# Two edits to a kernel of attention and two expert layers: a wait of the gathers of noise is left out, and one piece of TensorE's work is put behind a vote

## The reference

```
x  = attention(q, k, v)            # 4 x 8 heads x 768, chunks of 32 keys with 16 to the left, 8 to the right, 8 memory keys
x  = moe(x)                        # 3072 tokens, 8 experts, capacity 384 each

def _moe_ref(x, w_gate, w1, w2):
    logits = x @ w_gate
    order = np.argsort(-logits.flatten())
    for idx in order:              # the best (token, expert) pairs first
        tok, e = idx // E, idx % E
        if assigned[tok] >= 0 or counts[e] >= cap: continue
        assigned[tok] = e; counts[e] += 1
    for e in range(E):
        out[assigned == e] = relu(x[assigned == e] @ w1[e]) @ w2[e]

def _moe2_ref(x, w_gate, w_noise, noise, w1, w2):
    noisy = x @ w_gate + log1p(exp(x @ w_noise)) * noise
    # the best two experts of each token, weighted by the softmax of their two values
    # out += weight * (relu(x @ w1[e]) @ w2[e])
```

## Time and profile before

| | |
|---|---|
| median of 3 runs | 1321.05 us (1320.45 to 1321.9) |
| profiled execution, its own time | 1320.45 us |
| its span | 1318.6 us |
| TensorE's mean granted clock | 0.969 of full speed |
| busy, of the span | PE 93%, DVE 69%, ACT 43%, POOL 22% |

### The profile page before, as it was taken

How to read it: one execution, slowest core, us unless ns; L and a number is a source line. 1 busy time by engine, 2 the same in 40 slices (tenths; PEclk the granted TensorE clock), 3 DMA queues, 4 the chain that set the end, 5 groups by cost and what they waited for, 6 DMA issues and landing times.

```text
span 1318.6 us, 27799 instructions
## 1 busy us (share of the span) xinstructions
PE 1229.2 (93%) x9680; PEld 1094.3 (83%) x9680; DVE 915.5 (69%) x1818; ACT 572.2 (43%) x1224; POOL 291.1 (22%) x346
## 2 busy tenths in 40 slices
PE   6999983289999999999999999999999999999997
PEld 5888872278787787888898999989999898999986
DVE  4777765887887878765697666666666666766662
ACT  4666650123333233344415544544455444544541
POOL 4000000111211211220223323324233242333322
PEclk9999995589999999999999999999999999999999
DMA  8878744433331432543305233233333423334210
GB/s 147 167 169 166 167 100 175 152 113 108 126 121 64 146 128 73 176 156 121 110 28 198 72 106 111 81 104 106 126 122 121 144 79 104 100 125 135 88 43 13
DMA packets 174299, 154.65 MB, mean 117 GB/s; under 512 B 105118, under 2 KB 137886, under 8 KB 174241
## 3 DMA queue, kind: packets, MB, share of 16 engines
q1 hardware_dynamic: 151552, 102.83, 27.9%
q0 software_dynamic: 16128, 44.56, 10.9%
q10 hardware_dynamic: 6560, 6.49, 1.4%
HBM read 206.13 MB, written 33.75 MB: 182 GB/s over the span
## 4 chain that ended last, share of the span: by engine, by line
PE 38%; issue 36%; DVE 10%; POOL 9%; DMA 3%; ACT 2%; POOLq 1%; another core or an unknown queue 0%; SPq 0%; DVEq 0%; ACTq 0%
PE bank L792 8%; PE bank L772 8%; DMA out<-result,token_now 3%; POOL partial L424 3%; PE bank L648 3%; POOL out L434 3%; PE bank L657 2%; PE bank L636 2%; POOL held L404 2%; PE bank L1004 2%; PE bank L672 2%; POOL x L408 2%; PE bank L718 2%; PE bank L1031 2%; PE bank L757 1%
## 5 line engine op out<-in xcount | busy, mean ns | idle before, releaser
L575 DVE TENSOR_TENSOR w_part<-w_sb,w_part 128x1024 fp32r<-128x1024 f32 x280 | 341.6, 1223 | 98.0 <-ACT w_part L569 90.1
L569 ACT CAST w_part<-w_sb 128x1024 fp32r<-128x1024 f32 x280 | 290.6, 1046 | 205.9 <-PE bank L1031 152.5
L1004 PEld LDWEIGHTS bank<-x2T,w_part 128*128 128x128 f32 x2688 | 326.3, 192 | 4.4 <-DVE x2T L1561 1.4
L1004 PE MATMUL bank<-x2T,w_part 128*128 128x256 f32 x2688 | 327.9, 283 | 1.6 <-DVE x2T L1561 1.6
L1031 PE MATMUL bank<-w_part,h2T 128*128 128x512 f32 x1344 | 312.6, 391 | 0.0
L1031 PEld LDWEIGHTS bank<-w_part,h2T 128*128 128x128 f32 x1344 | 250.2, 188 | 51.0
L792 PE MATMUL bank<-w_part,hT 128*128 128x512 f32 x576 | 155.2, 406 | 3.7 <-DVE w_part L575 3.7
L772 PE MATMUL bank<-xgT,w_part 128*128 128x384 f32 x768 | 147.0, 344 | 0.9 <-DVE xgT L1225 0.9
L1916 ACT ACTIVATE h2T<-bank 128x512 fp32r<-128x512 f32 x112 | 66.9, 597 | 178.6 <-PE bank L1004 141.1
L772 PEld LDWEIGHTS bank<-xgT,w_part 128*128 128x128 f32 x768 | 134.1, 191 | 2.9 <-DVE xgT L1225 1.4
L1567 DVE SCALAR_TENSOR_TENSOR h2T<-bank,h2T 128x512 fp32r<-128x512 f32 x112 | 77.3, 690 | 79.9 <-ACT h2T L1916 55.8
(11 more groups left out here) (281 smaller groups left out, 1337.2 us busy)
## 6 DMA issues: line engine op xcount, KB each, us to landing
w_sb<-in_moe_w SPq DMA_DIRECT2D x280, 512.0 KB
k_in<-in_k SPq DMA_DIRECT2D x32, 240.0 KB
v_in<-in_v SPq DMA_DIRECT2D x32, 240.0 KB
q_in<-in_q SPq DMA_DIRECT2D x32, 192.0 KB
x_dram<-x_sb SPq DMA_DIRECT2D x32, 192.0 KB, 3.2
out<-zeros SPq DMA_DIRECT2D x1, 6144.0 KB, 19.7
y_dram<-y_sb ACTq DMA_DIRECT2D x24, 256.0 KB, 2.0
x<-y_dram,slot_now POOLq DMA_INDIRECT x56
```

What stands on the lines that cost most here:

```text
L569: scalar.copy(split_part(0, c), raw_part(c)).then_inc(hi_ready[c], 1)
L575: nc.vector.tensor_tensor(split_part(1, c), raw_part(c), split_part(0, c).bitcast(F32), ALU.subtract).then_inc(lo_ready[c], 1)
L1004: last = nc.tensor.matmul(bank[2 + g % 2][:, at:at + TILE], w1_part[a][:, kt, f * P:(f + 1) * P], x2T[b][:, kt, :], start=(f % 2 == 0 and ...
```

## The change

```diff
@@ -379,9 +379,6 @@
                     pool.indirect_dma_start(out=xg[:, c % TPE, :], out_offset=None, in_=x_dram[:, :],
                                             in_offset=bass.IndirectOffsetOnAxis(ap=token_of[:, c:c + 1], axis=0),
                                             bounds_check=N - 1, oob_is_err=False).then_inc(gathered[c % TPE], 16)
-                if e < E - 2:
-
-                    pool.wait_ge(s1_ready, e * FT + 6)
                 for c in range(e * TPE, (e + 1) * TPE):
                     pool.indirect_dma_start(out=noise_g[:, c, :], out_offset=None, in_=moe2_noise[:, :],
                                             in_offset=bass.IndirectOffsetOnAxis(ap=token_of[:, c:c + 1], axis=0),
@@ -806,8 +803,8 @@
 
             def step(n, k, j):
 
-                before_votes = (0, 6, 9, 12, 15, 20, 22)
-                after_votes = (3, 8, 11, 14, 17, 21, 24)
+                before_votes = (0, 6, 9, 12, 15, 18, 22)
+                after_votes = (3, 8, 11, 14, 17, 20, 24)
                 done = 0
                 for s in range(len(SHIFTS)):
                     count(n, s)
```

## The result

| | before | after |
|---|---|---|
| median, on the chip on which both were first timed | 1320.81 us (4 runs, 1320.45 to 1321.90) | 1329.26 us (4 runs, 1327.67 to 1332.73) |
| ratio, with its 95% interval | | 1.0063 [1.0047, 1.0079] |
| profiled execution, its span | 1320.45, 1318.6 us | 1327.07, 1325.2 us |
| TensorE's mean granted clock | 0.969 | 0.966 |

The kernel is slower by 0.6%, 8.4 us, where 1320.1 us and "no difference that can be told" were forecast. The time is outside the forecast's range (1318.0 to 1322.3), and a slower kernel was given 6%.

A forecast was written before the change was run, and what follows sets the result against it. VectorE was taken to set the pace early in each step, TensorE from 402.20 to 421.80 in step 4. Terms -0.96 + 0.05 + 0 = -0.9 us, from 1321.05 to 1320.1 us; range 1318.0 to 1322.3.

The forecast's parts named there:

- The second edit, gain: Combine pieces moved from ahead of vote 5 to ahead of vote 6: vote 5 earlier, vote 6 unmoved, gain 0.
- Rival A: VectorE's 2.25 us idle before vote 5 is on the path: 1.41 us gained in five steps, 1313.1 us; 8%.
- The second edit, cost: Vote 5 behind three matmuls instead of nine still comes 0.6 us after VectorE's comparison: no new wait, cost 0.
- The first edit, cost in steps 2 to 6: Noise gathers in their new place hold VectorE up by at most 0.3 us, hidden in its slack: cost 0.
- Rival B: The 0.28 us gap ahead of the first comparison is due to gathers: 1.1 us more gain, 1319.0 us; 7%.
- The first edit, gain: Noise gathers leaving each step's start free VectorE's small instructions, shortening TensorE's weight-block wait: 0.96 us over steps 2 to 6.
- Step 1: No combine there, VectorE on the path: moved gathers may hold up L1359, bounds 0 to 0.3 us, taken as 0.05.
- Rival C: First gathered block lands too late for the earlier transposes: up to 1.41 us lost in five steps, 1327.2 us; 6%.

The follow-up runs named there:

- E2: Kernel before with only the combine pieces moved, noise gathers waiting as before: 1320.17 us, ratio 1.0000.
- E9: Kernel before with only the combine pieces moved, repeated on another chip: 1320.64 us, ratio 1.0006.
- E16: Kernel before with only the combine pieces moved, repeated to mark the chip's kind: 1320.98 us, ratio 1.0006.
- E18: Kernel before with only the combine pieces moved, on a chip with late signals: 1321.88 us, ratio 1.0002.
- E17: Kernel before with only the noise gathers moved up behind those of xg, on a chip with late signals: 1319.17 us, ratio 0.9977.
- E6: Kernel before, unchanged, profiled on a chip without late signals: 1320.77 us, ratio 1.0002.
- E1: Kernel before with only the noise gathers moved up behind those of xg, combine pieces as before: 1318.84 us, ratio 0.9993.
- E5: Kernel after, unchanged, on a chip without late signals: 1319.55 us, ratio 0.9990.
- E14: Kernel after, unchanged, run as a marker of the chip's kind: 1320.02 us, one run.
- E7: Kernel after, unchanged, a third time on yet another chip, which showed late signals: 1327.39 us, ratio 1.0052.
- E4: Kernel after without the third noise gather of the first six expert places, that noise zero: 1320.12 us, ratio 0.9997.
- E13: Kernel before with only the noise gathers moved up behind those of xg, repeated: 1320.60 us, ratio 1.0002.
- E8: Kernel before with only the noise gathers moved up behind those of xg, repeated: 1319.00 us, ratio 0.9992.
- E11: Kernel after, noise gathers of six places replaced by 2 KB rows of x, their noise zero, repeated: 1367.15 us, ratio 1.0358.
- E12: Kernel before with only the noise gathers moved up behind those of xg, repeated: 1319.38 us, ratio 0.9989.
- E3: Kernel after, noise gathers of the first six places replaced by 2 KB rows of x, their noise zero: 1367.14 us, ratio 1.0359.
- E10: Kernel after without the third noise gather of the first six places, that noise zero, repeated: 1320.09 us, ratio 0.9997.

## Why the prediction was wrong, point by point

**The second edit, gain.** Right. That VectorE's 2.25 us of idleness ahead of delta was not on the path is borne out by E2, E9, E16 and E18: the step keeps its length (51.45 against 51.46, 51.67 against 51.70). Rival A is out. The three matmuls and the vote that I read at 408.92 and 409.81 are those of s = 4, not of s = 3 as the earlier trace rows and the forecast say; the 0.89 us between them stand.

**The second edit, cost: "still 0.6 us behind the comparison, so no new wait is made".** This is the step that failed, together with the next. The 0.6 us were worked out with the comparison ready at 413.25, as early as it is in the earlier trace rows with no gather beside it. In the same change the first edit puts gathers beside it. The comparison was taken as fixed, when it was the one thing that the other edit could move.

**The first edit, cost in steps 2 to 6: "It would vanish in either slack. Cost in steps 2 to 6: 0".** I bounded the hold-up by the longest instruction beside a gather, 0.3 us, and asked only what a gather does to an instruction that runs. What goes with it on chips of the first kind is a late signal, by 1.8 us at s = 5. That is three times the slack of 0.63 us (413.88 - 413.25), and what is left over, 1.78 - 0.63 = 1.15 us, is about the wait that was measured (1.11 us there, 1.11 to 1.16 in the five steps). It costs 5.7 us in waits, and 3.0 us by the clock behind two of them. Before the change the slack there was 2.04 us (415.29 - 413.25), which covers 1.8 (E17): the second edit was counted as free because nothing waited, and it took away the cover that the first edit needed.

**Rival B.** It was the warning, and I argued it away. On the chip of the first runs the gap ahead of the first comparison does belong to the gathers: it goes when they go (after: 1.14 us behind the weight block, where the earlier trace rows has 1.42), and E6 shows 1.15 with gathers and no late signal. My two reasons against it fail. "Step 2 has the gathers and not the gap": the signal there is late too, by the semaphore's record (the matmul ends at 284.77, the signal is at 285.57), and the weight block hides it. "Register work is the nearer cause": E6 has the same register work and no gap. With 0.18 us marked "remote" and a block of 1.2 us just ahead, what is seen is the end of a wait whose beginning is covered; the count had ended 1.5 us earlier. Read so, it prices the lateness at about 1.5 us in a row of before, and the new place has cover for 0.6.

**The first edit, gain: 0.96 us.** About right in its own terms: the chain takes 2.79 or 2.80 us in all steps of after, and no instruction there is held up. On the other kind of chip the step shortens by 0.25 us, some 1.2 us over five steps; on the first kind by 0.47, since the gap's 0.28 us go as well, which is rival B's extra gain. The step was forecast at 51.5 us and is 51.2 in E17. One sign failed: TensorE's wait for the low weight block did not shrink from 0.76 us.

```profile
399.65 1.63 PE L789 MATMUL bank<-w_part,hT 128*128 128x512 f32 x6 [0.76 <-DVE w_part L572]
```

It is the other wait of the earlier trace rows that the gain came off, TensorE's 0.45 us for the table of s = 1, which the forecast named and did not use. In after it is gone, as in E17:

```profile
395.76 0.76 PE L715 MATMUL bank<-proposal,above 128*32 128x8 bf16 x24
```

In E6 that wait is 0.23 us and in E1 it is gone. So the wait that is used up is about as long as the gain of the step, on both kinds.

**Step 1: +0.05.** Right within its bounds. L1356 at 259.82 takes 0.29 us, so the last gather does not hold it up, and step 1 to 2 is shorter than before by 0.42 us.

**Rival C.** Out: the transposes have no wait for a transfer in after or E5. The rival on the slower side was the wrong one. Its time, 1327.2 us, is near the 1327.07 of the profiled execution by luck: it lost 1.41 us in five steps to a late block, the kernel loses 1.1 in five to a late signal and 1.5 in two to the clock, less what it gains.

**The range.** It held what this program does on the one chip of E5 and E14 (1319.55 and 1320.02). It did not hold its time on the chips of the first result and of E7, because no case of the forecast had one edit remove the cover of another.

## What stays open

Why the signal is late on some chips and not on others with the same instructions is not known; of the chips met, those of the first result, of E7 and of E17 and E18 show it, and four others (E1 to E4; E5, E6, E13 to E16; E8 to E11; E12) do not. Which chip gave the first result is not on record; it may be one of the other two. The chip of E5 was met on three occasions and was of the other kind on all three; the chips of the first kind were met on one occasion each, so that it is the chip and not the occasion is likely, not shown. What in a gather makes the signal late is open: the number of gathers and what they read were not varied on a chip of the first kind, since E3, E4, E10 and E11 met none. The half clock came behind two of five waits in after and two of five in E7, and no trace has one between 275 and 637 us without such a wait (E3, E5, E10 and E13 have one or two in the last layer, from 638 us on); which of the waits brings it can't be forecast from these runs, nor how much of the spread of after, 1327.67 to 1332.73 us, comes of it.

## What to carry to other kernels

Two edits that are each free can cost something together: price each edit's slack with the other one in place, and ask of every filler between a producer and its consumer what lateness it covers, not only whether somebody waits there now. A small unexplained wait ("remote", 0.18 us) right behind a long instruction is the visible end of a longer one: take the distance from the true producer's end, and use that as its price. And when a small loss does not come back on another chip, compare the kernel before with itself on both chips before explaining the kernel.

## What the runs showed of the hardware

In the first result and on the chips of E7 and E17, semaphore signals of TensorE reached VectorE 1.5 to 1.8 us late in the loop's steps, when the matmul ended 0.1 to 0.6 us into an indirect gather of noise by GpSimd (rows of 32 bytes); on the four others they came within 0.05 us in the same place. On the same chips a signal to ScalarE was late beside a gather of 2 KB rows of `out` (0.86 us at 736.25 in before), and signals beside the gathers of 2 KB rows of `x_dram` were not (0.01 us). TensorE's own work went on at its usual pace meanwhile (2.37 us for nine matmuls in E17). An idle time of TensorE of 1.1 us was followed by 3.4 us at 1.2 GHz in four of the ten cases of after and E7, at a price of 1.5 us each in after. A VectorE instruction is held up by up to 0.26 us beside a noise gather on both kinds of chips (L1162: 0.44 us in step 2 of before and 0.43 in E6, 0.18 elsewhere), so this is a thing apart from the late signal.
